# Gate logits of the routing summed head by head inside the attention, as extra columns of the matrix that turns its outputs

## The reference, cut to what matters

```python
scores = q @ k.T / 8 + bias(i, j, head)                 # 4 batches, 8 heads, 576 rows, head size 64
attn   = softmax(scores) @ v
x      = attn, heads side by side                       # 2304 tokens x 512
logits = x @ w_gate + modality_bias[modality_id]        # w_gate: 512 x 8 experts
expert = argmax(logits); weight = softmax(logits)[expert]
y      = weight * (relu(x @ w1[expert]) @ w2[expert])   # w1: 512 x 1024, w2: 1024 x 512
out    = max(y @ a, y @ b, y @ c) @ w_out
```

## Time and profile before

| | us |
|---|---|
| median of three executions | 987.44 |
| the profiled execution, whole | 985.97 |
| its span, first to last instruction | 983.9 |
| bias stage, to the first scores of the heads' loop | 60.4 |
| attention, to its last PE operation | 60.4 to 317.9 |
| routing, to the first gather | 322.6 to 349.7 |
| experts and the final layers | to 983.9 |
| busy: PE, DVE, ACT, POOL | 885.5, 544.7, 341.8, 334.9 |

### The profile page before, as it was taken

The page is one execution under the profiler, slowest core; times in us unless marked ns, Lnnn a source line. Parts: engine busy times, 40 slices in busy tenths (PEclk is TensorE's granted clock), DMA queues, the critical chain, the costliest instruction groups (busy, mean ns, idle before and its releaser), DMA issues.

```text
span 983.9 us, 25115 instructions
## 1 busy us (share of the span) xinstructions
PE 885.5 (90%) x9890; PEld 761.4 (77%) x9890; DVE 544.7 (55%) x1007; ACT 341.8 (35%) x728; POOL 334.9 (34%) x290
## 2 busy tenths in 40 slices
PE   6867788778777659999999999999999999999998
PEld 3446666667666637888888888889999999999997
DVE  7977788889884494444444575445423333323331
ACT  7965476676764613411000131133211110111100
POOL 0618654231321469954000484487420202010100
PEclk9977799999999869999999999999999999999999
DMA  4687786777853667743000354354320102000001
GB/s 163 241 253 215 181 218 185 196 187 182 210 128 96 218 192 256 213 151 107 22 23 22 118 175 137 118 160 127 110 65 1 65 1 65 1 33 2 33 1 32
DMA packets 70464, 120.55 MB, mean 123 GB/s; under 512 B 26632, under 2 KB 29864, under 8 KB 68344
## 3 DMA queue, kind: packets, MB, share of 16 engines
q1 hardware_dynamic: 47320, 73.65, 26.0%
q10 hardware_dynamic: 17616, 30.27, 10.3%
q0 software_dynamic: 5456, 15.60, 5.0%
HBM read 92.58 MB, written 26.90 MB: 121 GB/s over the span
## 4 chain that ended last, share of the span: by engine, by line
PE 60%; POOL 5%; issue 1%; DVE 1%; ACT 0%; ACTq 0%; POOLq 0%
PE moe_banks L1505 23%; PE moe_banks L1460 12%; PE moe_banks L1426 12%; PE moe_banks L1522 8%; POOL slots L1194 3%; PE moe_banks L1444 2%; PE moe_banks L1363 1%; POOL x_behind L1204 1%; PE moe_banks L1411 1%; POOL x_tok L1204 1%; PE moe_banks L1488 1%; PE moe_banks L1372 1%; POOL x_tok L1232 0%; DVE in_lane L1607 0%; ACT x_tok L1324 0%
## 5 line engine op out<-in xcount | busy, mean ns | idle before, releaser
L1194 POOL TENSOR_TENSOR slots<-x_tok,slots 128x512 fp32r<-128x512 f32 (+1 forms) x116 | 140.9, 1254 | 155.8 <-ACT slots L1302 155.5
L1505 PE MATMUL moe_banks<-yT,slots 128*128 128x384 f32 x1080 | 193.1, 334 | 0.0
L1505 PEld LDWEIGHTS moe_banks<-yT,slots 128*128 128x128 f32 x1080 | 188.0, 188 | 0.5
L1302 ACT CAST slots<-x_tok 128x512 fp32r<-128x512 f32 (+1 forms) x116 | 67.9, 602 | 257.9 <-PE moe_banks L1426 128.6
L1426 PE MATMUL moe_banks<-slots,xT 128*128 x600 | 146.5, 400 | 4.5 <-ACT slots L1302 2.3
L1460 PE MATMUL moe_banks<-slots,hT 128*128 x600 | 140.3, 389 | 0.6 <-POOL slots L1194 0.6
L729 ACT ACTIVATE probs<-probs,negmax 128x576 f32<-128x576 f32 x144 | 110.8, 770 | 75.7 <-DVE negmax L680 75.0
L1426 PEld LDWEIGHTS moe_banks<-slots,xT 128*128 128x128 f32 x600 | 113.0, 192 | 29.0 <-issue 5.6
L1460 PEld LDWEIGHTS moe_banks<-slots,hT 128*128 128x128 f32 x600 | 112.6, 188 | 24.1 <-issue 0.8
L680 DVE CUSTOM_DVE_ANT_0 probs<-s_ps,bias 128x576 f32<-128x576 f32 x144 | 103.3, 750 | 41.9 <-PE s_ps L591 38.5
L591 PE MATMUL s_ps<-kT,qT 64*128 64x288 f32 x768 | 75.7, 331 | 45.9 <-DVE negmax L680 36.1
(11 more groups left out here) (175 smaller groups left out, 994.5 us busy)
## 6 DMA issues: line engine op xcount, KB each, us to landing
x_tok<-in_moe_w ACTq DMA_DIRECT2D x96, 256.0 KB, 3.0
v_raw<-in_v SPq DMA_DIRECT2D x64, 288.0 KB, 5.5
bias_table<-staged SPq DMA_DIRECT2D x36, 296.0 KB, 3.2
bias<-bias_table SPq DMA_DIRECT2D x32, 288.0 KB, 3.8
result_rows<-y SPq DMA_DIRECT2D x25, 256.0 KB, 2.2
q_raw<-in_q SPq DMA_DIRECT2D x16, 320.0 KB, 3.7
k_raw<-in_k SPq DMA_DIRECT2D x16, 288.0 KB, 3.3
x_rows_by_tile<-x_tok SPq DMA_DIRECT2D x16, 288.0 KB, 3.4
```

The lines of the kernel that those rows point to most:

```text
L1194: nc.gpsimd.tensor_tensor(rest, raw(n, rows), near.bitcast(F32), ALU.subtract).then_inc(part_done(e, part)[0], 1)
L1302: nc.scalar.copy(near, raw(n, rows)).then_inc(near_done, 1)
L1505: last = nc.tensor.matmul(u_ps[m], final_weight(far, slots, m, d, a, f), yT[:, c, d, :], start=(d == 0 and k == 0), stop=(d == KD - 1 and ...
```

## The change

Each head's part of the logits is made in the attention. The identity with which `outputs` turns gets eight (for the shared tile) or sixteen further columns, the 64 rows of w_gate of that head for either batch; so the five transposes become five float32 products, four of 144 columns and one of 136. ACT copies these columns aside in two further copies ahead of its four. POOL scales them by the same sums (three multiplications) and adds them to the logits, ahead of its scaling of the outputs; the logits begin as the modality bias. The widened identity (eight heads of it, 152 columns a head) is loaded by three SP loads behind the keys and queries of head 1, and PE waits for all three where it waited for the identity. The second turning of `x_tok`, the gate products, their copies and the addition on DVE go. SP's two groups of loads wait for the stored rows of each pair alone. At the tail one part of the values' products moves ahead of the outputs of unit 14.

```diff
+GATE = 2 * EXPERTS
+TURNED = GATE + P
...
+        turn_gate = sb("turn_gate", [P, HEADS, TURNED + EXPERTS])
...
             for u in range(2):
                 load_values(sp, 0, u)
                 keys_queries(sp, 1, u)
+                if u == 0:
+                    sp.dma_start(turn_gate[:, :, GATE:TURNED],
+                                 identity_dram.unsqueeze(1).broadcast_to([P, HEADS, P])).then_inc(turn_gate_in, 16)
+                    sp.dma_start(turn_gate[:, :, 0:GATE], w_gate[:, :, 0:GATE]).then_inc(turn_gate_in, 16)
+                    sp.dma_start(turn_gate[:, :, TURNED:], w_gate[:, :, GATE:]).then_inc(turn_gate_in, 16)
...
+            def add_gate(it, u):
+                n = unit(it, u)
+                pool.wait_ge(gate_copied, n + 1)
+                pool.wait_ge(gate_added, n + 1)
+                for b in range(2):
+                    tiles = slice(b * (COMB + 1), b * (COMB + 1) + FULL)
+                    nc.gpsimd.tensor_tensor(gate_part[:, tiles, :], gate_raw[:, :, b * EXPERTS:(b + 1) * EXPERTS],
+                                            inv[:, u, tiles].unsqueeze(2).broadcast_to([P, FULL, EXPERTS]), ALU.mult)
+                nc.gpsimd.tensor_tensor(gate_part[:, COMB, :], gate_raw_shared[:], inv[:, u, COMB:COMB + 1].broadcast_to([P, EXPERTS]),
+                                        ALU.mult).then_inc(gate_scaled, 1)
+                pool.wait_ge(gate_scaled, n + 1)
+                logits = routing["logits"][:, u * TILES:(u + 1) * TILES, :]
+                nc.gpsimd.tensor_tensor(logits, logits, gate_part[:], ALU.add).then_inc(gate_added, 1)
+
             def scale_outputs(it, u):
                 pool.wait_ge(inv_done, unit(it, u) + 1)
+                add_gate(it, u)
                 pool.wait_ge(x_copied, unit(it, u) + 1)
...
                 for tile in range(FULL + 1):
-                    to = x_ps[0][:, tile * P:(tile + 1) * P] if tile < FULL else x_ps[1]
-                    last = nc.tensor.transpose(to, out_T[:, tile * P:(tile + 1) * P], ident[:])
+                    to = x_ps[:, tile // 2, tile % 2, :] if tile < FULL else x_ps_shared
+                    last = nc.tensor.matmul(to, out_T[:, tile * P:(tile + 1) * P], turn_gate_of(it, tile), start=True, stop=True)
                 last.then_inc(x_filled, 1)
...
             pe.wait_ge(bias_sems["evacuated"], BIAS_STEPS)
-            pe.wait_ge(ident_in, 16)
+            pe.wait_ge(turn_gate_in, 48)
             pe.wait_ge(zeroed, 1)
             heads_loop(pe, head)
+            values(HEADS - 1, 1, VALUES[0])
             pe.wait_ge(x_copied, unit(HEADS - 1, 0))
             outputs(HEADS - 1, 0, FULL * unit(HEADS, 0))
-            values(HEADS - 1, 1, range(KEY_BLOCKS))
+            values(HEADS - 1, 1, range(VALUES[0].stop, KEY_BLOCKS))
...
             def copy_output(it, u):
-                act.wait_ge(x_filled, unit(it, u) + 1)
+                n = unit(it, u)
+                act.wait_ge(x_filled, n + 1)
+                if not (isinstance(n, int) and n == 0):
+                    act.wait_ge(gate_scaled, n)
+                nc.scalar.copy(gate_raw[:].rearrange("p (k t) e -> p k t e", k=2), x_ps[:, :, :, 0:GATE])
+                nc.scalar.copy(gate_raw_shared[:], x_ps_shared[:, P:]).then_inc(gate_copied, 1)
...
-            sp.wait_ge(x_stored, 16 * PAIRS * HEADS)
-            sp.wait_ge(turned, HALF_LOADS)
+            sp.wait_ge(x_stored[0], 16 * HEADS)
             for n, (rows, _, _) in enumerate(half_group(1, 0)):
                 sp.dma_start(raw(n, rows), rows).then_inc(chunk_in[n], 16)
-            sp.wait_ge(turned, 2 * HALF_LOADS)
+            sp.wait_ge(x_stored[1], 16 * HEADS)
...
-            for t in range(0, T, 2):
-                turned_out(t)
-                n = t // 2
-                if n < HALF_LOADS:
-                    act.wait_ge(stage_in[n % SHORT_RING], 16 * (n // SHORT_RING + 3))
-                    nc.scalar.copy(half_group(0, 0)[n][1], stage[:, n % SHORT_RING, :]).then_inc(near_done, 1)
+            for n, (_, near, _) in enumerate(half_group(0, 0)):
+                act.wait_ge(stage_in[n % SHORT_RING], 16 * (n // SHORT_RING + 3))
+                nc.scalar.copy(near, stage[:, n % SHORT_RING, :]).then_inc(near_done, 1)
...
-            for q in range(QUADS):
-                for t in quad(q):
-                    turn(t)
-                if q:
-                    gate(q - 1)
-            gate(QUADS - 1)
...
-            dve.wait_ge(gate_turned, 1)
-            nc.vector.tensor_tensor(logits[:], logit_of, tok_bias[:], ALU.add).then_inc(routed, 1)
+            nc.vector.memset(chosen[:, T, :], 0.0).then_inc(routed, 1)
             dve.wait_ge(routed, 1)
```

More of the change, by code:

```diff
@@ L246, in lay_out @@
     arrays["k"] = np.ascontiguousarray(by_dimension(arrays["k"])).reshape(PAIRS, HEADS, P, SEQ)
+    gate = np.zeros((2, DH, HEADS, 3, EXPERTS), np.float32)
+    for b in range(2):
+        gate[b, :, :, b, :] = gate[b, :, :, 2, :] = arrays["moe_w_gate"].reshape(HEADS, DH, EXPERTS).transpose(1, 0, 2)
+    arrays["moe_w_gate"] = gate.reshape(P, HEADS, 3 * EXPERTS)
     values = arrays["v"].reshape(PAIRS, 2, HEADS, KEY_BLOCKS, HIDDEN, DH).transpose(0, 2, 4, 1, 3, 5)
@@ L290, in build_attention @@
         out_T = sb("out_T", [P, (FULL + 1) * P])
[L292 removed]
+        turn_gate_in = sem("turn_gate_in")
+        gate_copied, gate_scaled, gate_added = sem("gate_copied"), sem("gate_scaled"), sem("gate_added")
         zeroed = sem("zeroed")
@@ L375, in token_bias @@
             pool.wait_ge(tok_bias_made, 4)
-            nc.gpsimd.tensor_tensor(routing["tok_bias"][:], bias_of[:, 0], bias_of[:, 1], ALU.add)
+            nc.gpsimd.tensor_tensor(routing["logits"][:], bias_of[:, 0], bias_of[:, 1], ALU.add).then_inc(gate_added, 1)
         VALUE_LOADS = 16 * QUADRANTS
@@ L533, in _ @@
             nc.gpsimd.memset(one[:], 1.0).then_inc(one_set, 1)
-            routing["zero"](pool)
             nc.gpsimd.memset(inv[:], 0.0).then_inc(x_scaled, 1)
@@ L755, in copy_output @@
                     first = u * TILES + b * (COMB + 1)
-                    nc.scalar.copy(x_tok[:, first:first + FULL, head],
-                                   x_ps[0].rearrange("p (t b d) -> p t b d", b=2, d=DH)[:, :, b, :])
+                    nc.scalar.copy(x_tok[:, first:first + FULL, head].rearrange("p (k t) d -> p k t d", k=2),
+                                   x_ps[:, :, :, GATE + b * DH:GATE + (b + 1) * DH])
                 for b in range(2):
                     part = slice(b * REM, (b + 1) * REM)
-                    last = nc.scalar.copy(x_tok[part, u * TILES + COMB, head], x_ps[1][part, b * DH:(b + 1) * DH])
+                    last = nc.scalar.copy(x_tok[part, u * TILES + COMB, head], x_ps_shared[part, b * DH:(b + 1) * DH])
                 last.then_inc(x_copied, 1)
@@ L976, in load @@
                     put(inputs["mod_id"][p0:p0 + rows.shape[0], pair * TILES + tile, :], rows)
-        eng.wait_ge(inputs["gate_zeroed"], 1)
-        put(inputs["gate_w"][:, :, 0:E], w_gate.rearrange("(k p) e -> p k e", p=P))
-    inputs["zero"], inputs["load"] = zero, load
+    inputs["load"] = load
     return inputs
@@ L990, in build_moe @@
     T, E = ALL_TILES, EXPERTS
-    QUADS = -(-T // 4)
     ring = x_tok
-    gate_w, ident, tok_bias, half = (inputs[name] for name in ("gate_w", "ident", "tok_bias", "half"))
+    ident, logits, half = (inputs[name] for name in ("ident", "logits", "half"))
     below, powers, total, total_eps = softmax
@@ L1003, in build_moe @@
         y = [sb(f"y{r}", [P, MODEL]) for r in range(2)]
-        x_T = over("x_T", [P, 2, 4, MODEL])
-        again = area(nc, base)
-        in_tile = again("in_tile", [P, T, SLOT_TILES])
-        id_in_tile = again("id_in_tile", [P, T, SLOT_TILES], F16)
-        in_lane = again("in_lane", [P, T, P], F16)
-        gate_T = over("gate_T", [P, QUADS * P])
-        logits = over("logits", [P, T, E])
+        in_tile = over("in_tile", [P, T, SLOT_TILES])
+        id_in_tile = over("id_in_tile", [P, T, SLOT_TILES], F16)
+        in_lane = over("in_lane", [P, T, P], F16)
+        over.end[0] = SMALL_TABLES + base
         top = over("top", [P, T])
```

90 lines of the change are left out of this document (25 added, 65 removed).

## The result

The kernel after took 1002.99 us (median of four executions, 1001.18 to 1005.96) where the kernel before took 988.16 (four, 986.79 to 993.44): ratio 1.0143, 95% interval 1.0095 to 1.0191. The profiled execution took 1001.3 us with a span of 999.5, 15.6 over the span before. The sign held, and the time lies inside the range. But the centre, 1014, was 11 us too high: a change of +28 us was forecast, and +15 was measured.

The account below looks back on a forecast made before the run. After the routing PE's products bound the kernel; before, a unit is one chain of outputs, ACT's copies, next scores and DVE without slack. 985.97 + 17.0 + 17.1 + 2.3 - 8.0 = 1014.4 us, range 997 to 1028.

Parts of the forecast that it names:

- The start stall, +17.0: At the heads' loop start, PE waits for three loads of the widened identity until 77.4, losing 17.0 us (13.1 to 19).
- The output step, 13.5 units at 1.27: Each loop unit: five products +0.87 us, ACT's two copies +0.40, together 1.27; over 13.5 units +17.1 us (12.8 to 23).
- rival 1: In the loop units, DVE rather than PE's scores sets the pace and absorbs the output step; 993 us, chance 0.10.
- Rival 2: In the output step, products cost 4.5 times the turning, 2.84 us, +2.6 a unit with ACT; 1035 us, chance 0.05.
- The tail, +2.3: Behind the loop, two output steps on PE's path, ACT's copies and POOL's operations add 2.3 us (1.8 to 3.2).
- The routing, -8: Between the meeting and PE's third tile, DVE reduces logits earlier; the third tile gains 8 us (ends -3 and -15.2).
- The first step of the argument: In the routing, POOL's eight subtractions for expert 0 lie beside DVE's chain; first gather 15.2 us earlier at best.
- The step on SP's loads and ACT's and DVE's subtractions for expert 1: Routing: SP's loads, then DVE's subtractions for expert 1, end 8 to 3 us earlier; third tile gains 5.3 to 10.5.
- The collision with the gathers: In the routing, eight gathered rows run beside SP's weight loads for expert 1, delaying them by up to 5.3 us.
- Rival 3: In the routing, gathers collide with the weight loads and only 3 us come back; 1019 us, chance 0.07.
- The mutual hold of DVE and POOL: In the routing, DVE's chain beside POOL's subtractions could lose up to 10 us, the sum rising up to 6; left out.
- Rival 4: At the loop's start, the widened identity's loads are there before PE asks; 997 us, chance 0.04.

Follow-up runs that it names:

- Experiments 1 to 3: Kernel after with the three loads issued first, 997.7 us; kernel after with PE's wait one head later, 998.88 us; kernel before with late load alone, 1012.28 us.
- experiment 10: Kernel before with its five transposes an output step made ordinary float32 products with the same 128-column identity; 998.20 us, ratio 1.0077.
- wide products (4): Kernel before with its five transposes made float32 products of 144 and 136 columns, the extra columns unread zeros; 1001.91 us, ratio 1.0094.
- wide products, two copies (6): Kernel before with products of 144 and 136 columns and ACT's two further copies, to buffers nobody reads; 1003.38 us, ratio 1.0093.
- experiment 3: Kernel before with its identity loaded late in three loads of the widened shapes, PE waiting for all, transposes kept; 1012.28 us, ratio 1.0188.
- experiment 7: Kernel after with POOL's eight subtractions for the first expert made to wait for DVE's routing chain; 1017.37 us, ratio 1.0236.
- experiment 1: Kernel after with the three loads of the widened identity issued right behind head 0's keys and queries; 997.7 us, ratio 1.0058.

## Why the prediction came out as it did

**The start stall, +17.0.** Right in mechanism, and in size on the first chip (+16.4). Experiments 1 to 3 show it alone, taken away in two ways and put in by itself. The arrival was right partly by luck: I took 4.0 us behind the keys' landing, a middle between two paces of the queue, and did not see the 5.14 us that the third issue costs. (The high end was also mis-added: 73.42 + 5.5 is 78.9, a loss of 18.5 and not 19.) On other chips it was 18.1 to 21.6, partly over my upper end.

**The output step, 13.5 units at 1.27.** The term that was mis-sized. The nine steady units of each trace, split by the granted clock (a unit's time is the mean of those at that clock):

| kernel | outputs to next scores | a unit at clock 1.00 | a unit at 0.89 | units at 0.89, of nine |
|---|---|---|---|---|
| before | 2.02 | 14.57 | 15.21 | 3 |
| plain products (experiment 10) | 2.59 | 15.11 | 15.77 | 5 |
| wide products (4) | 2.69 | 15.19 | 15.86 | 5 |
| wide products, two copies (6) | 2.78 | 15.30 | 15.95 | 6 |
| after | 2.77 | 15.30 | 15.97 | 6 |

So the step costs 0.73 us a unit at one and the same clock: 0.62 the products and 0.11 the copies, against 0.87 and 0.40. The other 0.21 of the measured 0.96 stands for units that run partly at the lower clock, which I had not in the sum at all. Why there are more of them is not shown. It is not the products alone: experiment 3, with transposes, has five of nine. For the copies I added durations (0.22 and 0.18) where the pace between starts is what counts, 0.11 and 0.06; I had the remark on PE's pace at hand and did not apply it to ACT. The products' estimate of 0.30 us each was high because I took the values' products as like; 0.26 was measured, near my lower end of 0.245 from the bias products' column pace. DVE was never the bound (rival 1): its idle time doubled. Rival 2 is out: an ordinary product is twice a transpose in this place (0.24 for 128 columns against 0.126), not four times. The Trainium skill (TensorE: Matmul & The Clock Gate, Terms) gives the factor of four; the runs here show 1.9, and the measurement decides. A product's two instructions take 0.12 us each to the next start, and a transpose's one takes 0.126.

**The tail, +2.3.** +1.5 in the first pair of traces, below its lower end of 1.8. Two output steps at the 0.75 us between outputs and next scores are 1.5, so by this estimate the same mis-sized term explains it.

**The routing, -8.** -11.0; the further -1.6 behind the third tile is the clock, which I had not foreseen. The first step of the argument, that the chain of DVE and the eight subtractions of POOL lie side by side, was right; but the subtractions ended 3.5 us ahead of `source`, and the first gather came 16.55 us behind the meeting, later than the 12 to 15 of the forecast. The step on SP's loads and ACT's and DVE's subtractions for expert 1 failed. I had made them the bound of the third tile (8 to 3 us earlier). The new kernel's DVE finished them at 373.1, 22.3 us behind the meeting, and took up its first gathered rows at 22.8, against 32.4 in the kernel before (355.04): 9.7 us earlier. What held DVE last was then the gather, by 0.48 us. The collision with the gathers, for which I had put in up to 5.3 us, did not come: all sixteen loads were issued before the first gather was. Rival 3 (only 3 us given back) is out. On B and C less comes back than on A, 5.5 to 8.3 us: the third tile starts 58.1 to 59.8 us behind the meeting in the kernels with the new routing (without experiment 7, at 63.8), and 65.2, 66.4 and 67.0 us with the old (experiments 3, 4 and 6).

**The mutual hold of DVE and POOL,** which I mentioned and left out of the sum, is real and cost 5.7 us of the chain. The trace agrees with the rule of the Trainium skill (SBUF — State Buffer, Who interferes with whom) on operations with two SBUF inputs: experiment 7 has the same operation at 0.96 us without POOL and 1.98 with it. The case that I had quoted for it, 1.27 us at 383.03, did not show that rule: it is a TENSOR_SCALAR with one SBUF input. The hold did delay the first gather, by about 3.5 us as an estimate (`source` at 366.42, POOL free from 362.92). For the first tile leaving it out of the sum was near enough, but not for a reason that I had given: ACT's casts for expert 1 ran to 372.34 and DVE's subtractions behind them to 373.07, so a gather without the hold could have brought DVE to its rows only about 0.5 us earlier. Putting the subtractions behind the chain made nothing faster.

**Rival 4,** loads that land before PE asks, is out by the stall.

**What the errors did.** The heads' loop 17.1 to 10.3, routing -8 to -11.0, tail and stall -1.4, the clock in the third tile 0 to -1.6: all on the same side, 12.8 us together, and that is the difference between the sum and the measured trace, 1014.4 to 1001.3, within 0.3. Of the loop's 6.8 us the mis-sized unit explains 4.2 (0.31 times 13.5); the other 2.6 are in its first and last units and stay open. That the time fell inside the range is owed to the range's width, 31 us, and not to the size of the terms. On chip C, where the change cost 19.8 us, the forecast's 28 was too high too.

## What to carry to other kernels

A matrix that the very first step of a loop's body waits for, though only a later one uses it, should be waited for where it is used: one line moved was worth some 9 to 14 us here (1.0056 on B, against 1.0143 on A and 1.0199 on C; the two were never run on one chip). When a short operation is added to a dense chain, price it by the distance between starts in like rows and not by its duration. A transpose turned into a true float32 product doubled the instructions and their weight loads, at 128, 136 and 144 columns alike. And where PE's pace differs between two traces, look at the granted clock of just that stretch: an average of 1.00 over the last 600 us hid 0.77 over the 7.3 us that made the difference.

## What I had not expected of the hardware

- The third of three loads of 1,024 pieces each held SP's queue for 5.14 us in the kernel after and for 4.86 to 5.25 in five further traces, the first two for 0.43 and 0.60 to 1.04, though the third had the least data. At the front of the stream (experiment 1) the three took 0.43, 1.91 and 4.32. If it is the 32-byte pieces or the pieces still under way, no run tells apart.
- DVE's casts of a few elements from SBUF to SBUF, with one input, were held by POOL just as those with two: 18 elements a lane 1.06 us instead of 0.18, eight elements 1.23 instead of 0.17.
- The same program took 11.3 us on A and 20.4 on C between its first two tiles of the experts.
- A unit of the same work lasts 0.65 us longer when the granted clock falls to 0.50 inside it, and whether it does changes from unit to unit: three of nine in the kernel before, six of nine in the kernel after.
